# Turned loops of VectorE and ScalarE, a fourth row buffer, and an earlier end of GpSimd's stream in the second of two expert mixtures

## What is computed

```python
do_compute = x @ w_skip > 0
out = x.copy()
xc = x[do_compute]
logits = xc @ w_gate
e_idx = np.argmax(logits, axis=1)
gate_w = softmax(logits)[chosen expert]
for e in range(E):
    mask = e_idx == e
    h = np.maximum(xc[mask] @ w1[e], 0.0)
    y[mask] = gate_w[mask, None] * (h @ w2[e])
out[do_compute] = xc + y
```

## Time and profile before

| what | value |
|---|---|
| time, median of 3 executions | 811.5 us (811.49, 811.5, 812.82) |
| the profiled execution: time / span of its trace | 811.92 us / 810.2 us |
| second mixture: first matmul of tile 0, last matmul of tile 10 | 653.97 us, 801.15 us |
| tiles in this execution | 11, with 7 changes of expert |
| busy share of the span: TensorE, VectorE, ScalarE, GpSimd | 94%, 43%, 32%, 9% |
| mean granted clock of TensorE | 0.97 of full speed |

### The profile page before, as it was taken

The page is one execution under the profiler, slowest core; times in us unless marked ns, Lnnn a source line. Parts: engine busy times, 40 slices in busy tenths (PEclk is TensorE's granted clock), DMA queues, the critical chain, the costliest instruction groups (busy, mean ns, idle before and its releaser), DMA issues.

```text
span 810.2 us, 12852 instructions
## 1 busy us (share of the span) xinstructions
PE 758.3 (94%) x4497; PEld 665.8 (82%) x4498; DVE 349.2 (43%) x817; ACT 260.6 (32%) x570; POOL 73.2 (9%) x114
## 2 busy tenths in 40 slices
PE   5679989999999999999999999999999779899995
PEld 4468888888998998989989899898989657678774
DVE  4767564452442221244212144213224479754961
ACT  3645444351320100123101032020204147744751
POOL 2331000000000000000000000001010244221220
PEclk9769999999999999999999999999999979999998
DMA  9694622112211000033000022121121448961920
GB/s 200 155 203 103 133 61 57 38 35 104 98 61 50 1 0 0 0 104 104 0 0 0 0 84 72 52 78 40 39 79 68 171 161 308 330 248 39 324 88 17
DMA packets 77321, 75.02 MB, mean 93 GB/s; under 512 B 54484, under 2 KB 54740, under 8 KB 76896
## 3 DMA queue, kind: packets, MB, share of 16 engines
q1 hardware_dynamic: 74224, 69.82, 28.8%
q0 software_dynamic: 3056, 4.66, 1.9%
HBM read 67.77 MB, written 9.29 MB: 95 GB/s over the span
## 4 chain that ended last, share of the span: by engine, by line
PE 84%; issue 4%; DVE 4%; DMA 4%; ACT 1%; DVEq 1%; POOL 0%; POOLq 0%; ACTq 0%; SPq 0%
PE ps L1152 26%; PE ps L1154 25%; PE ps L1153 25%; PE ps L1186 2%; PE ps L1214 1%; DMA out_rows<-acc,first_ids 1%; PE ps L1314 1%; DVE w_lo L876 1%; PE ps L1200 1%; PE ps L1165 1%; DMA acc<-x_rows,id_of 1%; DMA acc<-stage 1%; PE ps L1304 1%; PE ps L1383 1%; DVE acc L836 1%
## 5 line engine op out<-in xcount | busy, mean ns | idle before, releaser
L1152 PE MATMUL ps<-w_hi,h_hi 128*128 128x512 f32 x472 | 188.4, 399 | 4.9 <-DVE h_lo L1101 4.8
L1154 PE MATMUL ps<-w_hi,h_lo 128*128 128x512 f32 x472 | 184.5, 391 | 0.0
L1153 PE MATMUL ps<-w_lo,h_hi 128*128 128x512 f32 x472 | 184.3, 390 | 0.0
L663 ACT ACTIVATE h_hi<-ps 128x384 fp32r<-128x384 f32 x128 | 63.0, 492 | 367.3 <-PE ps L1154 367.2
L1152 PE MATMUL ps<-xt_hi,w_hi 128*128 128x384 f32 (+1 forms) x512 | 175.6, 343 | 2.5 <-issue 2.4
L1154 PE MATMUL ps<-xt_hi,w_lo 128*128 128x384 f32 (+1 forms) x512 | 172.3, 337 | 0.0
L1153 PE MATMUL ps<-xt_lo,w_hi 128*128 128x384 f32 (+1 forms) x512 | 172.3, 336 | 0.0
L881 DVE SCALAR_TENSOR_TENSOR h_lo<-ps,h_hi 128x384 fp32r<-128x384 f32 x128 | 71.2, 556 | 177.3 <-ACT h_hi L663 177.1
L1152 PEld LDWEIGHTS ps<-w_hi,h_hi 128*128 128x128 f32 x472 | 88.7, 188 | 24.3 <-DVE h_lo L1101 6.7
L1154 PEld LDWEIGHTS ps<-w_hi,h_lo 128*128 128x128 f32 x472 | 88.6, 188 | 19.0
L1153 PEld LDWEIGHTS ps<-w_lo,h_hi 128*128 128x128 f32 x472 | 88.8, 188 | 16.8
(11 more groups left out here) (170 smaller groups left out, 679.6 us busy)
## 6 DMA issues: line engine op xcount, KB each, us to landing
stage<-in_moe_w SPq DMA_DIRECT2D x56, 512.0 KB, 4.5
acc<-in_moe_w SPq DMA_DIRECT2D x36, 512.0 KB, 6.0
stage<-in_k SPq DMA_DIRECT2D x16, 192.0 KB, 4.3
acc<-in_v SPq DMA_DIRECT2D x4, 768.0 KB, 6.9
x_rows<-acc SPq DMA_DIRECT2D x4, 768.0 KB, 3.6
out_rows<-acc SPq DMA_DIRECT2D x4, 768.0 KB, 5.2
acc<-in_moe_w POOLq DMA_DIRECT2D x4, 512.0 KB, 5.4
v_all<-in_v SPq DMA_DIRECT2D x16, 120.0 KB, 2.8
```

The costliest lines, as they stand in the source:

```text
L663: nc.scalar.activation(h_hi[:, f, :], ps[:, f % 2, 0:GT], ACT.Relu).then_inc(h_hi_ok, 1)
L1152: mm(dst, a_hi, b_hi, start=start, stop=False)
L1153: mm(dst, a_hi, b_lo, start=False, stop=False)
L1154: return mm(dst, a_lo, b_hi, start=False, stop=stop)
```

## The change

Three things. First, the bodies of the VectorE and ScalarE loops are turned: a body for tile i now ends with the first half of h of tile i+1 (`relu_h(i+1,0)`, `high_h(i+1,0)`, `low_ht(i+1,0)`), so that the turn of the loop, with its two register loads, stands behind that half and not ahead of it. Where the expert changes, ScalarE does `relu_h(i+1,0)` ahead of the last w2 piece, and VectorE does `low_ht(i+1,0)` between the second and the third w2 piece. The two cases (change of expert or not) become the two sides of an `If ... Else`. TensorE ends with two transposes, so that the half of h past the last tile has something to wait for. Second, there are four row buffers, and the second layer's sums alternate between two PSUM banks. Third, the wait for the last scatter moves from GpSimd to SyncE. The tests `i < tiles` are nested within a round, and SyncE gets a row of the table of its own, which costs one more small VectorE operation behind the table.

```diff
-    SLOTS = 3
+    SLOTS = 4
@@ sync
-            sp.wait_ge(table_ok, 1)
+            sp.wait_ge(from_ok, 1)
...
+            sp.wait_ge(scattered, 16 * tiles)
+            hold(sp, "sp")
@@ gpsimd
-            gate(2, fetch(2, 2))
+            for i in range(2, SLOTS):
+                gate(i, fetch(i, i))
...
-                        with gp.If(i + 1 < tiles):
-                            gate(k, fetch(i + SLOTS - 1, k))
-                        scatter(i, (k + 1) % SLOTS, ...)
-            gp.wait_ge(scattered, 16 * tiles)
-            hold(gp, "pool")
+                        gate(k, fetch(i + SLOTS - 1, k))
+                        scatter(i, at, id_of[:, at:at + 1])
+                        if k + 1 < SLOTS:
+                            turn(k + 1)
@@ scalar, loop over i
-                    relu_h(i, 0)
-                    high_h(i, 0)
                     relu_h(i, 1)
                     split_x(i + 1)
-                    high_h(i, 1)
                     with act.If(now < then):
+                        high_h(i, 1)
                         split_w1(then + E1, slots1)
-                        next_w2(i, then)
+                        next_w2(i, then, range(PIECES - 1))
+                        relu_h(i + 1, 0)
+                        next_w2(i, then, range(PIECES - 1, PIECES))
+                        high_h(i + 1, 0)
+                    with act.Else():
+                        high_h(i, 1)
+                        relu_h(i + 1, 0)
+                        high_h(i + 1, 0)
@@ vector
+            nc.vector.tensor_scalar(table[:, 1 + 3 * TAB:1 + 4 * TAB], ...).then_inc(from_ok, 1)
@@ vector, loop over i
-                        low_ht(i, 0)
                         low_x(i + 1)
                         low_ht(i, 1)
                         with dve.If(now < then):
-                            low_w1(then + E1, lambda j: stage[:, j, :])
-                        rows_out(i, (k + 1) % SLOTS)
-                        with dve.If(now < then):
-                            for c in range(PIECES):
-                                low_w2(then + E1, c, stage2[:, c, :])
+                            lows_w1(then)
+                            rows_out(i, at)
+                            lows_w2(then, range(PIECES // 2))
+                            low_ht(i + 1, 0)
+                            lows_w2(then, range(PIECES // 2, PIECES))
+                        with dve.Else():
+                            rows_out(i, at)
+                            low_ht(i + 1, 0)
@@ tensor
-                    last = three(ps[:, 5 + k, :], h_hi[:, f, 0:P], ...)
+                    last = three(ps[:, 5 + k % 2, :], h_hi[:, f, 0:P], ...)
...
+            nc.tensor.transpose(ps[:, 0, 0:P], ident[:, :], ident[:, :]).then_inc(r1_done, 1)
+            nc.tensor.transpose(ps[:, 2, 0:P], ident[:, :], ident[:, :]).then_inc(ht_done, 1)
```

More of the change, by code:

```diff
@@ L568, in _, with turn @@
             with gp.Fori(0, ROUNDS) as r:
-                for k in range(SLOTS):
-                    i = SLOTS * r + k + 1
+                def turn(k):
+                    i, at = SLOTS * r + k + 1, (k + 1) % SLOTS
                     with gp.If(i < tiles):
@@ L746, in high_h, with next_w2 @@
                                      ACT.Copy).then_inc(ht_hi_ok, 1)
-            def next_w2(i, then):
-                for c in range(PIECES):
+            def next_w2(i, then, pieces):
+                for c in pieces:
                     act.wait_ge(r2_done, PIECES * i + c + 1)
@@ L762, in _ @@
             relu_h(0, 1)
-            high_h(0, 1)
             with act.If(now < then):
+                high_h(0, 1)
                 split_w1(then + E1, slots1, range(PIECES // 2))
-            split_x(1)
-            with act.If(now < then):
+                split_x(1)
                 split_w1(then + E1, slots1, range(PIECES // 2, PIECES))
-                next_w2(0, then)
+                next_w2(0, then, range(PIECES - 1))
+                relu_h(1, 0)
+                next_w2(0, then, range(PIECES - 1, PIECES))
+                high_h(1, 0)
+            with act.Else():
+                high_h(0, 1)
+                split_x(1)
+                relu_h(1, 0)
+                high_h(1, 0)
             with act.Fori(1, TILES) as i:
@@ L1117, in _, with lows_w1, lows_w2, turn @@
             then = dve.value_load(table[0:1, 2 + 2 * TAB:3 + 2 * TAB], min_val=0, max_val=E2 - 1)
+            def lows_w1(then, pieces=range(PIECES)):
+                low_w1(then + E1, lambda j: stage[:, j, :], pieces)
+            def lows_w2(then, pieces):
+                for c in pieces:
+                    low_w2(then + E1, c, stage2[:, c, :])
             low_ht(0, 0)
[L1119 removed]
             with dve.If(now < then):
[L1121 to L1128 removed]
+                low_ht(0, 1)
+                lows_w1(then, range(PIECES // 2))
+                low_x(1)
+                lows_w1(then, range(PIECES // 2, PIECES))
+                rows_out(0, 0)
+                lows_w2(then, range(PIECES // 2))
+                low_ht(1, 0)
+                lows_w2(then, range(PIECES // 2, PIECES))
+            with dve.Else():
+                low_ht(0, 1)
+                low_x(1)
+                rows_out(0, 0)
+                low_ht(1, 0)
             with dve.Fori(0, ROUNDS) as r:
[L1130 to L1131 removed]
+                def turn(k):
+                    i, at = SLOTS * r + k + 1, (k + 1) % SLOTS
                     with dve.If(i < tiles):
@@ L1138, in _ @@
                         with dve.If(now < then):
-                            low_w1(then + E1, lambda j: stage[:, j, :])
-                        rows_out(i, (k + 1) % SLOTS)
-                        with dve.If(now < then):
-                            for c in range(PIECES):
-                                low_w2(then + E1, c, stage2[:, c, :])
+                            lows_w1(then)
+                            rows_out(i, at)
+                            lows_w2(then, range(PIECES // 2))
+                            low_ht(i + 1, 0)
+                            lows_w2(then, range(PIECES // 2, PIECES))
+                        with dve.Else():
+                            rows_out(i, at)
+                            low_ht(i + 1, 0)
+                        if k + 1 < SLOTS:
+                            turn(k + 1)
+                turn(0)
         @block.tensor
```

46 lines of the change are left out of this document (22 added, 24 removed).

## The result

| | kernel before | changed kernel |
|---|---|---|
| time beside each other, median (lowest to highest of 5) | 812.82 us (811.49 to 814.13) | 807.83 us (806.49 to 808.43) |
| ratio, 95% interval | | 0.9934 [0.9912, 0.9956] |
| the profiled execution: time / span of its trace | 811.92 / 810.2 us | 808.43 / 806.7 us |
| mean granted clock of TensorE | 0.972 | 0.968 |

What follows compares the result with a forecast made beforehand. TensorE bounds the kernel; only its second-mixture idle time and the end can be won. Stalls −8.9, ScalarE's turn +2.9 and the end −1.35 sum to −7.35 us from 811.5: 804.2 us, overall range 800.8 to 807.6.

Steps and rivals of the forecast that it cites:

- The order of views: Chain of waits first, then TensorE's waits, then its timeline: only TensorE's idle time in the second mixture and the end winnable.
- Stalls gone: TensorE's second-mixture waits for VectorE's low half of h and gathered rows vanish: −8.2 us, plus −0.7 at tile 1.
- ScalarE's turn: Loop branch, test and register loads between high_h and the second half's relu_h delay TensorE's transposes in ten tiles: +2.9 us.
- The price of 1.33 for each us: In TensorE's second mixture each us of shown idle costs 1.33 us, since the matmul pipeline empties and fills.
- The rival with the turn hidden: ScalarE's sequencer gets ahead in its loop, so TensorE waits nowhere new: 801.3 us; chance 0.12.
- What belonged to the gather: Tile 3's gather goes out in the prologue with four buffers, removing TensorE's 1.9 us wait, times 1.33, within 8.2 us.
- The jump: In ScalarE's loop, skipping the other side at six expert changes adds 0.2 us each; the skill's 51 ns was set aside.
- The DRAIN: GpSimd's closing DRAIN at the kernel's end starts about 1.4 us after the last scatter and lasts 3.9 us: −1.35 us.
- The rival in which it waits for the scatter: GpSimd's closing DRAIN waits for the scatter it follows and ends as late as before: 805.5 us; chance 0.14.
- Priced at nothing: Larger buffer memset, extra VectorE operation, three gathers of unused rows and two closing transposes lie beside waits or behind the last tile.
- The slower rival: Last two w2 pieces' loads land too late for ScalarE: 7.5 us lost at 9.0 us landing, 819.2 us at 10.5; chance 0.05.

Runs made afterwards that it cites:

- The repeats: The unaltered changed kernel measured two more times, each against the kernel before: 804.69 us, ratio 0.9919, and 806.16 us, ratio 0.9911.
- the repeat: The unaltered changed kernel run and traced once more, against the kernel before: 804.69 us, ratio 0.9919 [0.9898, 0.9940].
- the second trace of before: The kernel before, unaltered, run and traced once more: 813.12 us beside 812.02, ratio 1.0006; tile 1 to tile 10 second-layer starts 117.91 us.

## Why the prediction was right, and where a size was off

Forecast 804.2 us, or 0.991 of 811.5, with a range of 800.8 to 807.6. The first measurement, 807.83 us, lies 0.2 us above the range; beside the runs of before made with it (812.82) it is 0.9934, and on 811.5 that is 806.1 us. The repeats, 0.9919 and 0.9911, stand within 0.1% of the forecast.

- **The order of views** held: the time was to be won in TensorE's idle time in the second mixture and at the end, and in the repeat it came from there alone.
- **Stalls gone, and 2.9 us for ScalarE's turn** (−0.7, then −8.2 + 2.9 = −5.3 us): −0.87 and −5.47 us in the first trace; the repeat, against the same trace of before, −0.47 and −5.82. Both terms hold in the changed kernel itself. Nothing is left of the stalls in the long stretch, and what it has above nine periods of 12.30 us stands at `turn_h` alone: 2.7 us in the first trace and 2.4 in the repeat, where the nine tiles were forecast at 2.1 × 1.33 = 2.8. The price of 1.33 for each us held roughly: the repeat's 1.95 us of lateness in these tiles cost 2.4, 1.2 for each.
- **What the sum has no term for**: the two are not independent. Without ScalarE's turn the long stretch is 111.76 us and not 110.7, so taking the turn away wins 113.07 − 111.76 = 1.3 us and not 2.4. The prediction found VectorE's second half of h covered (732.8 for 733.5), but read this at a tile without a new expert. At a tile with one the two w2 pieces stand ahead of it, it ends 3.23 to 3.27 us behind M, and step f = 4 comes at 3.30 with ScalarE unturned. In the changed kernel ScalarE's lateness hides this, and that the sum needed no term for it is luck. The rival with the turn hidden, at 801.3 us, would have missed this 1.1 us.
- **What belonged to the gather** was mis-sized. I gave it 1.9 × 1.33 = 2.5 us of the 8.2. The trace of before without that wait in the loop is only 118.89 − 117.91 = 1.0 us shorter, since its wait lies where a stall for h stands anyway: seven waits for h instead of six. With three buffers 0.7 us of waiting came back. The 8.2 us suffer by it all the same, since they hold this 1.0 us of one trace: against the second trace of before the repeat wins about 6.7 us from the first matmul on (22.74 − 22.02 = 0.72 us up to tile 1, 4.84 in the long stretch and 1.2 behind it), less than the 7.35 forecast.
- **ScalarE's turn**: predicted late by 0.1 us in four tiles and 0.3 us in six, 2.2 us together. In the repeat `turn_h` was late by 0.03 to 0.07 us in the four, by 0.22 to 0.24 in four of the six, and by 0.47 and 0.40 in tiles 2 and 4, where a register load took 0.50 and 0.45 us: 2.0 us together. In the first trace it is 2.4 us, with tile 7 at 0.64, and one shown wait reached the 0.5 us that I had named as a bound. Periods were forecast at 12.4 to 12.7 us everywhere and are 12.40 to 12.82 in the repeat, 12.40 to 12.98 in the first trace.
- **The jump**: `relu_h` follows `high_h` by 1.75 us in tile 5 and by 1.90 us in tile 8 (766.31, 768.21), where the jump is added. That is 0.15 us, and the 0.2 that I took from the trace's own branch was the better price than the 51 ns of the Trainium skill (Advanced Engine Details and Errata, Control Flow Timing): what counts here is the time to the next instruction, not the length of the branch.
- **The DRAIN** (−1.35 us): it starts 1.4 us behind the scatter as predicted, but with the transfer in flight it takes 4.07 us, 0.16 more; −1.12 us from tile 10 on. The rival in which it waits for the scatter falls. The Trainium skill's 12 ns (VectorE: DVE Perf Modes, The DRAIN you can't avoid) isn't what this engine shows: VectorE, ScalarE and SyncE agree with it at 8 to 17 ns in both kernels, GpSimd doesn't. The page says it of the DRAINs that the runtime puts ahead of and behind a kernel; the profile puts these under a line of the kernel (L91), so they may be others.
- **Priced at nothing**: the larger memset. In the first trace it held VectorE up for 1.7 us, and the first matmul by about 0.9 us if the growth of the lateness is put down to it (3.0 us late ahead of it, 3.96 behind it). In the repeat, from the start of the memset to the first matmul are 654.04 − 644.62 = 9.42 us, before 653.97 − 644.65 = 9.32: 0.1 us.
- **The slower rival** (late w2 loads): in none of the waits of the changed kernel does TensorE or ScalarE stand behind such a load. A run that makes the loads later was not tried.

What the prediction left out is how far one trace stands from the next: the first matmul of the second mixture lay between 653.97 and 657.93 us over the fourteen traces of both kernels and their variants, a spread of 3.96 us, about half the gain.

## What to carry to other kernels

Cut two traces at the same places of the program before explaining a difference of spans: here about half of the gain was hidden by an earlier stretch, most of which the change doesn't touch, and a repeat removed it. A loop's turn has to stand where its engine waits anyway; at 1.7 to 2.1 us it fitted into none of the gaps between two operations of a half, and moving it from one gap to the next only changed which operand TensorE waited for. Check the slack of every operand that an edit moves at the tile where it is smallest: VectorE's second half was given 0.7 us at a tile without a new expert, and had 0.06 us at the tiles with one. Where two things end together, as the landing and the false tests at the end, neither alone is worth anything, so price them as a pair.

## What was not expected

- A register load of ScalarE from the same table took 0.28 us in most tiles and up to 0.70 us in some (0.76 in a variant), in the repeats in the same tiles (2, 4 and 7) or some of them. Why is open. The row of a body's first load in the first trace of the changed kernel (ns min/median/max):

```profile
L783 ACTq TENSOR_LOAD <-table x10: 276/286/695, 678.5 to 791.9; - x10
```

- Operations of VectorE beside GpSimd's memset are held in some places: a TENSOR_SCALAR and the TENSOR_REDUCE behind it 1.85 and 1.78 us for 0.17 once, and three TENSOR_SCALARs 1.02 to 1.04 us together for 0.68 in five runs with the memset of four buffers at its place, but not in the three where it was early. Others in the same memset kept their 0.18 us, and before, with the last 0.3 us of the smaller memset beside them, the three took 0.68 us. Why is open.
- TensorE's closing DRAIN, 8 ns in the kernels that end as before, took 1.50 us in the changed kernel (at 798.0), behind the two closing transposes. ScalarE's took 1.01 us with its loop unturned, where the closing `relu_h` and `high_h` are its last work. Nothing waited for either.
